# Key maxima and value sums of a block-sparse attention moved within set-up, with transposes ahead of them

## The chip, the core and the metric

The kernel runs on one core of a Trainium2 chip. The metric is the device time of one execution in microseconds, the median of three runs. Besides the program's span, from its first to its last instruction, an execution's time holds some 1.5 us around it. The engines are TensorE (PE), its weight load (PEld), VectorE (DVE), ScalarE (ACT), GpSimd (POOL) and SyncE (SP), which here only issues DMAs. TensorE's clock has two levels, 2.4 GHz (granted clock 1.00) and 1.2 GHz (0.50).

## The reference

Three stages follow each other: attention in 2 x 8 heads over 768 positions of width 64, a mixture of 8 experts with one expert per token, and a dense layer with a rational activation. Only the attention's set-up changes:

```python
block, window = (32, 16)
k_sum = k.reshape(B, H, nb, block, D).max(axis=3)      # block maxima of K
v_sum = v.reshape(B, H, nb, block, D).mean(axis=3)     # block means of V
scores_l = scale * np.matmul(q, k.transpose(0, 1, 3, 2))
mask_l = np.abs(pos[:, None] - pos[None, :]) < window
scores_s = scale * np.einsum('bhsd,bhnd->bhsn', q, k_sum) + np.log(block)
scores_all = np.concatenate([np.where(mask_l, scores_l, -1e9), scores_s], axis=-1)
a = softmax(scores_all)
out = np.matmul(a, np.concatenate([v, v_sum], axis=2))
```

Each position attends to the 31 keys around it and to the 24 block maxima of its head; the 24 block means of V stand beside the local values.

## The kernel before

Each engine runs its own program, written out by hand, and the programs meet in semaphores. An engine works in order, so a waiting instruction holds up all that is written behind it on its engine.

**Data.** 2 x 8 heads x 24 blocks make 384 block rows, three groups of 128 partitions (`KG` = 3). A row of `kraw` or `vraw` is one block of 32 positions x 64 elements, 1 MB per group. Groups 0 and 1 are needed for the first batch, group 2 with group 1 for the second.

**Set-up, keys.** SyncE loads `kraw` group by group (`load_k`, L366). ScalarE rounds each half of a group to the high part `KHL[HI]` (`key_halves`, L706), VectorE subtracts for the low part (`key_lo`, L964). TensorE transposes high and low side by side, four blocks of 128 columns per step, 8 steps per group, 24 in all (`key_columns`, L1341 is the line of every transpose). Step i writes bank i % 6, and may do so once step i - 6 has been copied out to `KTc`. ScalarE copies the steps (L713) but for steps 17, 19 and 21, which VectorE copies (`DVE_FILLS`, L970). VectorE makes the block maxima with a ladder of halving `max` operations over the row, in place in `kraw` (`key_max`, L977 the first step, L981 the four others), then splits the result into `KMX` (L983, L984). TensorE transposes `KMX` (`key_maxima`), ScalarE copies it to `KSs` (L717). Before, the maxima of groups 0 and 1 are made in set-up, those of group 2 in units 0 and 2 of the attention loop; TensorE's transpose of them stands at unit 4, into bank 7.

**Set-up, values.** TensorE sums each V group by matmuls with the identity into one bank (`value_sums`, L1357, banks 7 and 6), VectorE reduces the bank and scales (`mean_v`, L989, L990) and raises `vmean_ready`. SyncE stores the means to DRAM (L406), loads them back in the layout of `VA` (L402), and only then loads V's group 2 and query tile 2; GpSimd makes the third group's means with its own addition tree (`mean_v`, L522).

**Embedding.** ScalarE and VectorE normalise the expert embedding; TensorE transposes it; VectorE copies it (`place_embedding`, L957, L958), ahead of all its key work.

**GpSimd** makes `ident` (L472), then per query tile T: `split_q(T)` (high and low parts of the queries, L510 to L514) and `windows(T, half)` (gathers the keys of the tile from `KSs` and `KTc` into `KW`, L537, L539). `windows(0, 0)` waits for groups 0 and 1 of the columns and the first two maxima. Behind `windows(2, 1)` stand two loads of expert weights, the constants, and from tile 3 on, beside the tiles, the splitting of expert 0's weights in eight pieces (`split_slab0`, L549, L551: one piece with tile 3, two with 4, one with 5, two with 6, one each with 7 and 8) and indirect stores of x (L592).

**Attention loop.** 12 tiles x 4 head pairs = 48 units. Unit u on TensorE: `scores(u)` (L1424), `query_stack(u + 2)` (four transposes into bank 6 or 7), `transposes(u - 2)`, `products(u - 3)` (L1449, L1450). `query_stack(u)` with u % 4 == 0 waits for `split_q(u // 4)`. VectorE reduces scores to `es` (L1015) and copies `QS` for odd units (L1009), ScalarE does the exponentials (L742) and the even units' `QS` (L733).

The order of set-up on TensorE before:

```python
            embedding()
            key_columns(0)
            key_columns(1)
            key_maxima(0)
            value_sums(0)
            key_maxima(1)
            value_sums(1)
            key_columns(2)
```

## Time and profile before

| what | value |
|---|---|
| median of 3 runs (lowest, highest) | 752.04 us (751.38, 752.91) |
| the profiled execution: its time, its span | 747.03 us, 745.5 us |
| TensorE matmul busy | 684.3 us, 92% |
| VectorE, ScalarE, GpSimd busy | 500.2, 419.7, 171.9 us (67%, 56%, 23%) |
| chain that ended last, by engine | PE 76%, DMA 10%, DVE 5%, ACT 3% |
| mean granted TensorE clock | 0.97 |

The page cuts the span into 40 slices of 18.6 us; a digit is the busy share in tenths:

```profile
PE   4769999999387989999999999999999999999991
DVE  7576677676557468433411637899989899898881
POOL 4366999331331312111001000100000020200002
PEclk9989999999599999999999999999999999999997
```

The first three slices are set-up and the loop's first units, attention ends in the eleventh slice. TensorE is busy 4, 7 and 6 tenths there and 9 or more in the attention loop behind. GpSimd is nearly full in slices 5 to 7, and TensorE's clock is short of full in slice 3.

### The profile page before, as it was taken

Reading aid. Unit: us, or ns where it says so; the run is one execution under the profiler, and the core shown is the slowest. Engines: PE = TensorE matmul, PEld = TensorE weight load, DVE = VectorE, ACT = ScalarE, POOL = GpSimd, SP = SyncE. Lnnn points to the kernel's source line nnn. Section 1 sums busy time; section 2 is a strip of 40 time slices with the busy share of each in tenths; the row PEclk is TensorE's granted clock in tenths of the full one; section 3 lists DMA queues with packets and bytes.
Section 4 is the critical chain, followed back from the end, with each engine's and each line's share of the span. In section 5 each row is a group of like instructions: output and inputs, shape, how many; then the busy total and the mean of one; then the engine's idle time right before and its main releaser. Section 6 shows DMA issues by size and latency. Waiting matters only on the chain.

```text
span 745.5 us, 11775 instructions
## 1 busy us (share of the span) xinstructions
PE 684.3 (92%) x3397; PEld 547.3 (73%) x3397; DVE 500.2 (67%) x975; ACT 419.7 (56%) x786; POOL 171.9 (23%) x233
## 2 busy tenths in 40 slices
PE   4769999999387989999999999999999999999991
PEld 4457777777276777777888788888888888888871
DVE  7576677676557468433411637899989899898881
ACT  5445565565335577533523527777666666766650
POOL 4366999331331312111001000100000020200002
PEclk9989999999599999999999999999999999999997
DMA  8233544311698499823723440101000020100001
GB/s 295 56 93 113 135 131 109 79 47 45 212 325 252 139 308 323 276 59 105 265 84 100 142 157 15 57 0 30 15 14 1 1 71 1 42 15 1 0 1 56
DMA packets 52182, 77.75 MB, mean 104 GB/s; under 512 B 31680, under 2 KB 31696, under 8 KB 50840
## 3 DMA queue, kind: packets, MB, share of 16 engines
q1 hardware_dynamic: 43608, 51.51, 22.4%
q0 software_dynamic: 8064, 25.46, 10.3%
q8 instruction: 31, 0.51, 0.3%
q14 instruction: 31, 0.25, 0.1%
q10 hardware_dynamic: 448, 0.02, 0.1%
HBM read 63.50 MB, written 13.48 MB: 103 GB/s over the span
## 4 chain that ended last, share of the span: by engine, by line
PE 76%; DMA 10%; DVE 5%; ACT 3%; issue 2%; SPq 1%; POOL 1%; DVEq 1%; ACTq 0%; POOLq 0%
PE bank L1594 18%; PE bank L1609 17%; PE bank L1562 10%; PE bank L1341 10%; PE bank L1541 8%; DMA raw_late<-in_moe_w_dram 8%; PE bank L1450 4%; PE bank L1424 4%; PE bank L1449 3%; DVE weights L1206 2%; ACT weights L792 2%; DMA kraw<-in_k_dram 2%; PE bank L1469 1%; PE bank L1357 1%; DMA x_by_slot<-VA,zidx 1%
## 5 line engine op out<-in xcount | busy, mean ns | idle before, releaser
L1609 PE MATMUL bank<-weights,G 128*128 128x512 f32 x576 | 140.7, 393 | 1.9 <-DVE G L1206 1.9
L1594 PE MATMUL bank<-X2T,weights 128*128 128x512 f32 x576 | 141.1, 394 | 0.0
L1609 PEld LDWEIGHTS bank<-weights,G 128*128 128x128 f32 x576 | 108.1, 188 | 27.1 <-DVE G L1206 2.6
L1594 PEld LDWEIGHTS bank<-X2T,weights 128*128 128x128 f32 x576 | 107.5, 188 | 23.6
L1541 PE MATMUL bank<-weights,XT 128*128 (+1 forms) x456 | 116.9, 406 | 8.2 <-issue 4.0
L1562 PE MATMUL bank<-weights,HT 128*128 x456 | 112.6, 403 | 6.0 <-DVE HT L1206 6.0
L1541 PEld LDWEIGHTS bank<-weights,XT 128*128 128x128 f32 x456 | 85.3, 192 | 30.4 <-issue 11.8
L1562 PEld LDWEIGHTS bank<-weights,HT 128*128 128x128 f32 x456 | 85.7, 191 | 26.4 <-issue 7.1
L844 ACT ACTIVATE qd<-bank,coef 128x512 f32<-128x512 f32 x48 | 33.1, 689 | 73.5 <-PE bank L1594 73.4
L1206 DVE TENSOR_TENSOR HT<-bank,HT 128x512 fp32r<-128x512 f32 x38 | 24.5, 685 | 70.2 <-ACT HT L869 68.5
L742 ACT ACTIVATE es<-es,nmx 128x182 f32<-128x182 f32 x96 | 42.5, 444 | 25.5 <-DVE nmx L1015 25.5
L631 POOL DMA_DIRECT2D y_in_order<-yo x19 | 10.6, 557 | 200.2 <-ACT yo L896 200.2
L1206 DVE TENSOR_TENSOR weights<-raw_late,weights 128x2048 f32 (+1 forms) x20 | 41.4, 2077 | 22.4 <-ACT weights L792 22.4
L1206 DVE TENSOR_TENSOR weights<-raw_early,weights 128x2048 f32 (+2 forms) x20 | 40.6, 2075 | 15.5 <-ACT weights L792 15.2
L1256 DVE SCALAR_TENSOR_TENSOR qd<-sq,absb,qd 128x512 f32<-128x512 f32 x48 | 36.1, 751 | 21.1 <-ACT sq L845 21.1
L1015 DVE CUSTOM_DVE_ANT_0 es<-bank,mask 128x182 f32<-128x182 f32 x96 | 31.3, 344 | 22.5 <-PE bank L1424 22.0
L792 ACT CAST weights<-raw_late 128x2048 f32 x16 | 30.3, 1912 | 24.1 <-DMA raw_late<-in_moe_w_dram 24.1
L644 POOL DMA_INDIRECT out_dram<-ost,token_of x12 | 12.6, 1048 | 126.3 <-DVE ost L1244 123.3
L869 ACT CAST HT<-bank 128x512 fp32r<-128x512 f32 x38 | 20.4, 591 | 36.6 <-PE bank L1341 34.9
L852 ACT ACTIVATE pb<-bank,ncoef 128x512 f32<-128x512 f32 x48 | 37.9, 789 | 0.0
L1273 DVE SCALAR_TENSOR_TENSOR pb<-pb,ncoef,rr 128x512 f32<-128x512 f32 x48 | 36.1, 752 | 1.7
L1266 DVE SCALAR_TENSOR_TENSOR pb<-pb,ncoef,bank 128x512 f32<-128x512 f32 x48 | 35.9, 748 | 1.7
(215 smaller groups left out, 1156.1 us busy)
## 6 DMA issues: line engine op xcount, KB each, us to landing
raw_early<-in_moe_w_dram SPq DMA_DIRECT2D x14, 1024.0 KB, 8.2
raw_late<-in_moe_w_dram SPq DMA_DIRECT2D x14, 1024.0 KB, 10.3
y_in_order<-yo POOLq DMA_DIRECT2D x19, 256.0 KB, 3.2
x_all<-in_moe_w_dram POOLq DMA_DIRECT2D x8, 512.0 KB, 3.9
kraw<-in_k_dram SPq DMA_DIRECT2D x3, 1024.0 KB, 8.3
qraw<-in_q_dram SPq DMA_DIRECT2D x12, 256.0 KB, 4.1
x<-y_in_order POOLq DMA_DIRECT2D x12, 256.0 KB, 3.1
VA<-in_v_dram SPq DMA_DIRECT2D x10, 208.0 KB
```

Source lines behind the costliest of these rows:

```text
L742: A_.activation(e_, e_, ACT.Exp, bias=nmx[:, slot:slot + 1], scale=-1.0, accum_out=sums[:, T % 2, 2 * p + i:2 * p + i + 1]).then_inc(exp_d ...
L792: A_.copy(W[:, bass.ds(other, 1), HI, c * CH:(c + 1) * CH].rearrange("p s n -> p (s n)"), raw[c]).then_inc(half_hi[c // PER], 1)
L852: A_.activation(pb[s], h, ACT.Identity, bias=ncoef[:, 2:3], scale=ncoef[:, 3:4]).then_inc(lin_done, 1)
L1206: return V.tensor_tensor(out_, src, hi.bitcast(F32), ALU.subtract)
L1256: V.scalar_tensor_tensor(q_, h2, absb[:, 1:2], q_, ALU.mult, ALU.add).then_inc(q_done, 1)
L1266: V.scalar_tensor_tensor(g_, g_, ncoef[:, 1:2], h, ALU.add, ALU.mult).then_inc(h_read, 1)
L1273: V.scalar_tensor_tensor(g_, g_, ncoef[:, 0:1], r_, ALU.add, ALU.mult).then_inc(g_sb, 1)
L1341: return T_.transpose(dst, src, ident[0:rows, 0:rows])
L1541: last = T_.matmul(bank[half][:, :], XT[:, xa, kc * P:(kc + 1) * P], weights(par, wa, kc * F + half * BANK), start=(kc == 0 and n_ == 0), ...
L1562: last = T_.matmul(bank[5][:, :], HT[:, ha, fc * P:(fc + 1) * P], weights(par, wa, KC * F + fc * DM), start=(fc == 0 and n_ == 0), stop=(f ...
L1594: last = T_.matmul(bank[6 + f % 2][:, :], W[:, 0, wa, kc * F2 + f * P:kc * F2 + (f + 1) * P], X2T[c % 2][:, xa, kc * C_TOK:(kc + 1) * C_TO ...
L1609: last = T_.matmul(bank[tt][:, :], G[:, f % 2, ga, tt * P:(tt + 1) * P], W[:, 1, wa, f * DM:(f + 1) * DM], start=(f == 0 and n_ == 0), sto ...
```

## The change

SyncE issues the load of K's group 2 ahead of both V groups. VectorE's ladder for group 0 is no longer split around `key_lo(1)`, and the maxima of group 2 are made in set-up, behind `mean_v(0)` and ahead of the three key columns that VectorE copies; `mean_v(1)` goes behind those. All three maxima are transposed into bank 6, both value sums use bank 7 (so the second waits for `vmean_ready` 1), and TensorE's order becomes: 36 transposes of the identity into bank 7, embedding, 16 more, key columns 0 and 1, maxima 0, value sums 0, maxima 1, key columns 2, value sums 1, maxima 2. `query_stack(0)` waits for the third maxima's copy, `query_stack(1)` for the second means, and the loop for all 24 columns. ScalarE copies ten steps before it rounds group 2 instead of eight. The maxima leave the loop on all engines.

```diff
--- before.py
+++ after.py
@@ -408,9 +408,9 @@
             load_k(0)
             load_k(1)
             load_q(0)
+            load_k(2)
             load_v_all(0)
             load_v_all(1)
-            load_k(2)
             load_q(1)
             sp.wait_ge(cleared, 1)
             load_v(0)
@@ -706,25 +706,26 @@
                     A_.copy(KHL[:, g % 2, rows, HI, :],
                             kraw[:, g, :].rearrange("p (r d) -> p r d", d=D)[:, rows, :]).then_inc(k_hi, 1)
 
-            def key_columns(g):
-                for i in range(g * FILLS, (g + 1) * FILLS):
+            def key_columns(first, end):
+                for i in range(first, end):
                     if i not in DVE_FILLS:
                         act.wait_ge(kt_mm, i + 1)
                         A_.copy(kt_dst(i), kt_src(i)).then_inc(kt_act, 1)
 
             def key_maxima(g):
                 act.wait_ge(ks_mm, g + 1)
-                A_.copy(KSs[:, g * P:(g + 1) * P], bank[(6, 6, 7)[g]][:, g % 2 * P:(g % 2 + 1) * P]).then_inc(ks_sb, 1)
+                A_.copy(KSs[:, g * P:(g + 1) * P], bank[6][:, g * P:(g + 1) * P]).then_inc(ks_sb, 1)
 
             norm_of_embedding()
             key_halves(0)
             key_halves(1)
-            key_columns(0)
+            key_columns(0, FILLS + 2)
             key_halves(2)
-            key_columns(1)
+            key_columns(FILLS + 2, 2 * FILLS)
             key_maxima(0)
             key_maxima(1)
-            key_columns(2)
+            key_columns(2 * FILLS, KG * FILLS)
+            key_maxima(2)
 
             def query_stack(u):
                 act.wait_ge(q_mm, u + 1)
@@ -772,8 +773,6 @@
                     copy_pt(u - 2)
                 if u < UNITS:
                     exponent(u, 1)
-                if u == 4:
-                    key_maxima(2)
                 if u % 4 in (0, 2) and 4 <= u < UNITS + 4:
                     out_half(u // 4 - 1, u % 4 // 2)
                 if u % 4 == 1 and 9 <= u:
@@ -969,38 +968,34 @@
                 dve.wait_ge(kt_mm, i + 1)
                 V.tensor_copy(kt_dst(i), kt_src(i)).then_inc(kt_dve, 1)
 
-            def key_max(g, first, last):
+            def key_max(g):
                 t = kraw[:, g, :]
                 dve.wait_ge(k_lo, 2 * g + 2)
-                if first:
-                    w = ROW // 2
+                w = ROW // 2
+                while w >= D:
                     link(V.tensor_tensor(t[:, 0:w], t[:, 0:w], t[:, w:2 * w], ALU.max))
-                if last:
-                    w = ROW // 4
-                    while w >= D:
-                        link(V.tensor_tensor(t[:, 0:w], t[:, 0:w], t[:, w:2 * w], ALU.max))
-                        w //= 2
-                    link(V.tensor_copy(KMX[:, g, HI, :], t[:, 0:D]))
-                    V.tensor_tensor(KMX[:, g, LO, :], t[:, 0:D], KMX[:, g, HI, :].bitcast(F32), ALU.subtract)\
-                     .then_inc(kmax_ready, 1)
+                    w //= 2
+                link(V.tensor_copy(KMX[:, g, HI, :], t[:, 0:D]))
+                V.tensor_tensor(KMX[:, g, LO, :], t[:, 0:D], KMX[:, g, HI, :].bitcast(F32), ALU.subtract)\
+                 .then_inc(kmax_ready, 1)
 
             def mean_v(g):
                 dve.wait_ge(vm_mm, g + 1)
-                link(V.tensor_reduce(vmean[:, g, :], bank[7 - g][:, :].rearrange("p (r d) -> p d r", d=D), AX.X, ALU.add))
+                link(V.tensor_reduce(vmean[:, g, :], bank[7][:, :].rearrange("p (r d) -> p d r", d=D), AX.X, ALU.add))
                 V.tensor_scalar(vmean[:, g, :], vmean[:, g, :], 1.0 / BLOCK, None, ALU.mult).then_inc(vmean_ready, 1)
 
             scale_embedding()
             place_embedding()
             key_lo(0)
-            key_max(0, True, False)
             key_lo(1)
-            key_max(0, False, True)
-            key_max(1, True, True)
+            key_max(0)
+            key_max(1)
             key_lo(2)
             mean_v(0)
-            mean_v(1)
+            key_max(2)
             for i in DVE_FILLS:
                 key_column(i)
+            mean_v(1)
 
             def query_stack(u):
                 dve.wait_ge(q_mm, u + 1)
@@ -1112,8 +1107,6 @@
                     query_stack(u + 2)
                 if u % 4 in (0, 2) and 4 <= u < UNITS + 4:
                     out_half(u // 4 - 1, u % 4 // 2)
-                if u in (0, 2):
-                    key_max(2, u == 0, u == 2)
                 if u % 4 == 3 and u >= 7 and u < LOOPS - 1:
                     make_x(u // 4 - 1)
 
@@ -1352,9 +1345,9 @@
             def value_sums(g):
                 pe.wait_ge(v_all_in[g], 16)
                 if g == 1:
-                    pe.wait_ge(ks_sb, 2)
+                    pe.wait_ge(vmean_ready, 1)
                 for j in range(4):
-                    last = T_.matmul(bank[7 - g][:, :], ident[:, :], vraw[g][:, j * BANK:(j + 1) * BANK],
+                    last = T_.matmul(bank[7][:, :], ident[:, :], vraw[g][:, j * BANK:(j + 1) * BANK],
                                      start=(j == 0), stop=(j == 3))
                 last.then_inc(vm_mm, 1)
 
@@ -1377,21 +1370,25 @@
                 if g == 1:
                     pe.wait_ge(ks_sb, 1)
                 if g == 2:
-                    wait_qs(pe, 5)
-                transpose(bank[(6, 6, 7)[g]][:, g % 2 * P:(g % 2 + 1) * P], KMX[:, g, :, :].rearrange("p a d -> p (a d)").bitcast(F32))\
+                    pe.wait_ge(ks_sb, 2)
+                transpose(bank[6][:, g * P:(g + 1) * P], KMX[:, g, :, :].rearrange("p a d -> p (a d)").bitcast(F32))\
                     .then_inc(ks_mm, 1)
 
+            def warm_up(n):
+                for _ in range(n):
+                    transpose(bank[7][:, 0:P], ident[:, :])
+
+            warm_up(36)
             embedding()
+            warm_up(16)
             key_columns(0)
             key_columns(1)
             key_maxima(0)
             value_sums(0)
             key_maxima(1)
+            key_columns(2)
             value_sums(1)
-            key_columns(2)
-            wait_fills(pe, KG * FILLS)
-            pe.wait_ge(vmean_ready, 2)
-            pe.wait_ge(ks_sb, 2)
+            key_maxima(2)
 
             def query_stack(u):
                 T, p = divmod(u, PAIRS)
@@ -1401,8 +1398,10 @@
                     wait_qs(pe, u - 2)
                 if u % 4 == 2 and u >= 10:
                     pe.wait_ge(x_done, (u - 10) // 4 + 1)
-                if u == 7:
+                if u == 0:
                     pe.wait_ge(ks_sb, KG)
+                if u == 1:
+                    pe.wait_ge(vmean_ready, 2)
                 if u % 4 == 3 and u >= 11:
                     pe.wait_ge(lg_read, (u - 11) // 4 + 1)
                 for i in range(2):
@@ -1491,9 +1490,8 @@
 
             query_stack(0)
             query_stack(1)
+            wait_fills(pe, KG * FILLS)
             for u in range(LOOPS):
-                if u == 4:
-                    key_maxima(2)
                 if u % 4 == 0 and u >= 8:
                     if u >= 12:
                         if PAIRS * (u // 4 - 2) + 9 < UNITS:
```

## Rows read from the trace of the kernel before

**Rows 1.** Chain of waits, from the start: start us, length us, what.

```profile
5.79 14.17 DMA kraw<-in_k_dram
...
39.74 1.19 DVE kraw L977
```

**Rows 2.** Timeline of TensorE: start us, us, line, what, times [idle before it].

```profile
7.71 0.56 PE L1341 MATMUL bank<-ident,x_all 8*128 8x8 f32 x4 [7.71 <-DVE x_all L951]
10.08 8.79 PE L1341 MATMUL bank<-ident,KHL 128*128 128x128 f32 x56 [1.81 <-DVE KHL L964]
22.52 1.97 PE L1341 MATMUL bank<-ident,KHL 128*128 128x128 f32 x8 [3.64 <-ACT KTc L713]
...
29.11 3.67 PE L1357 MATMUL bank<-x_all,ident 128*128 128x512 f32 x8 [0.45 <-ACT KSs L717]
...
38.33 0.69 PE L1424 MATMUL bank<-KW,QS 128*128 128x182 f32 x4 [0.24 <-ACT QS L733]
...
50.49 0.44 PE L1341 MATMUL bank<-ident,KMX 128*128 128x128 f32 x1 [5.57 <-DVE QS L1009]
```

**Rows 3.** Timeline of VectorE.

```profile
15.56 2.81 DVE L981 TENSOR_TENSOR kraw<-kraw 128x512 f32<-128x512 f32 x4
...
20.03 1.74 DVE L981 TENSOR_TENSOR kraw<-kraw 128x512 f32<-128x512 f32 x4
...
28.59 0.69 DVE L989 TENSOR_REDUCE vmean<-bank 128x64 f32<-128x512 f32 x1 [4.07 <-PE bank L1357]
...
33.54 0.67 DVE L990 TENSOR_SCALAR vmean<-vmean 128x64 f32<-128x64 f32 x1
...
46.91 2.30 DVE L984 TENSOR_TENSOR KMX<-kraw,KMX 128x64 fp32r<-128x64 f32 x1
```

**Rows 4.** Windows: stretch, busy us (instructions) per engine, granted clock, DMA share, GB/s.

```profile
10.00:11.00 1.00, 0.92 (x5) 0.92 (x6) 1.00 (x2) 1.00 (x2) 0.00 (x0) 1.00 0.52 108
15.00:16.00 1.00, 1.00 (x11) 1.00 (x10) 1.00 (x2) 0.82 (x3) 1.00 (x1) 1.00 1.04 434
...
22.50:25.40 2.90, 2.88 (x11) 2.37 (x12) 2.02 (x2) 2.90 (x7) 0.00 (x0) 0.50 0.28 51
...
50.50:59.30 8.80, 8.80 (x32) 6.85 (x33) 3.20 (x13) 3.97 (x15) 7.74 (x22) 0.50 0.51 156
```

**Rows 5.** Timeline of SyncE's DMA issues.

```profile
2.43 2.56 SPq L371 DMA_DIRECT2D vraw<-in_v_dram  x1
...
37.00 0.42 SPq L377 DMA_DIRECT2D qraw<-in_q_dram  x1
```

**Rows 6.** DMA issues, 0 to 30 us: KB each, median us from issue to landing.

```profile
vraw<-in_v_dram SPq DMA_DIRECT2D x1, 1024.0 KB, 12.4
```

**Rows 7.** Timeline of GpSimd.

```profile
1.50 0.28 POOL L472 TENSOR_SCALAR_AFFINE_SELECT ident<-ident 128x128 f32<-128x128 f32 x1 [0.25 <-POOL ident L475]
...
14.53 2.25 POOL L514 TENSOR_TENSOR qhl<-qraw,qhl 128x512 fp32r<-128x512 f32 x1
...
42.82 0.61 POOL L510 CAST qhl<-qraw 128x512 fp32r<-128x512 f32 x1 [7.78 <-DMA qraw<-in_q_dram]
...
63.21 0.27 POOL L537 CAST KW<-KSs 128x96 fp32r<-128x96 f32 x1 [1.93 <-PE bank L1424]
63.42 0.71 POOL L539 CAST KW<-KTc 128x632 fp32r<-128x632 f32 x1
...
111.64 1.26 POOL L514 TENSOR_TENSOR qhl<-qraw,qhl 128x512 fp32r<-128x512 f32 x1
```

**Rows 8.** Instructions on tile kraw: duration ns min/median/max, first and last start us.

```profile
L964 DVE TENSOR_TENSOR KHL<-kraw,KHL x6: 1218/1222/1632, 8.8 to 23.3; 128x1024 fp32r<-128x1024 f32 x6
```

**Rows 9.** Timeline of TensorE, unit 26.

```profile
118.43 0.60 PE L1341 MATMUL bank<-ident,qhl 128*128 128x128 f32 x4
```

**Rows 10.** What TensorE waited for, 60 to 190 us: total, times, longest.

```profile
PE bank L1485 <- DVE oh L1068: 1.0, 1, 1.0
PE bank L1469 <- ACT OT L755: 0.4, 1, 0.4
```

## The prediction

> **What bounds the kernel now.** I read the page first, then the chain of waits, then each engine's timeline over the first 62 us, then the granted clock in windows of the same stretch. Through the attention loop the chain is TensorE's almost alone, so time saved in set-up reaches the end only if nothing else in the loop is nearly as late. The diff touches set-up and the loop's first steps; everything behind the loop is ordered by waits on its end, so I pass a shift on one for one.
>
> The start of the chain shows the two places the edit touches. K's third group lands at 5.79 + 14.17 = 19.96 us, behind both V groups [rows 1], and TensorE is idle from 18.87 (10.08 + 8.79) to 22.52. V's sums then run as one block, key columns follow, and the first scores come at 38.33 [rows 2]. In units 0 and 2 VectorE does the third group's maxima inside the loop; the last step ends at 46.91 + 2.30 = 49.21 [rows 3]. TensorE idles 5.57 us for it and restarts at 50.49 [rows 2]. It restarts slow: the granted clock is 0.50, the 1.2 GHz level, up to 59.3 at least [rows 4]. One trap: from 10 to 11 us the clock reads 1.00, the 2.4 GHz level, yet only 5 matmuls ran, and 11 in the us from 15 [rows 4]. The array was in fact slow until about 15 us, 4.9 us after the work at 10.08 began.
>
> **The loop's stall, the known gain.** With the maxima in set-up the loop loses the 5.57 us, the first maxima step in the chain (1.2, at 39.74), and what half clock costs: 8.8 us at half rate do the work of 4.4 [rows 1, 2, 4]. That is 11.2 us on TensorE's side, all on the path.
>
> **Load order.** The first V group, issued at 2.43, landed 12.4 later, at 14.8 [rows 5, 6]; K's third came 5.1 after that with one group between. The groups have one size and one queue, so I exchange the places: K's third at 14.8, V at 17.4 and 20.0. Nobody needs V before 19 (below). Cost nothing.
>
> **Warm-up.** The 36 transposes start when ident is ready, 1.78 [rows 7]. At half clock eight transposes took 1.97, some 0.22 each less the last one's tail [rows 2]; at full clock half of that. So they end at 9.7 all slow, 5.7 all fast, 8.2 with the rise after 4.9 us. The embedding's transposes started at 7.71 [rows 2], and VectorE's key work queues behind the copies that wait for them: 0 to 2 us on VectorE's chain, I take 0.5. The 16 later ones (1.8 us) fit before the first KHL halves. What warm-up brings is that the first 64 key transposes run at 0.11. They then are done well before VectorE has the maxima, so this gain is hidden.
>
> The Trainium skill (TensorE: Matmul & The Clock Gate, Part 4: PE-mode transpose) says that transposes don't count as work for the clock; the warm-up would do nothing. The trace disagrees: from 10.08 to 18.87 TensorE did transposes only, and their rate doubled near 15 [rows 2, 4]. By that rule the time would be the third rival's.
>
> **VectorE's chain decides set-up.** Up to the end of the second group's maxima its work is only permuted, and was without a gap; it ended 22.26, now 22.8. Then come, in the new order: key_lo(2), two of 1.22 [rows 8], to 25.2; mean_v(0), 0.93 (28.59 to 29.52) [rows 3], for which V's first sums (3.67 us [rows 2], from about 19.1) are on time; key_max(2), whose ladder takes 1.2 + 1.74 and the KMX steps 0.5, 3.4 clean [rows 1, 3]. Clean it ends at 29.5. But GpSimd works beside it. Beside its query split (its subtraction 2.25 instead of 1.26 us [rows 7]) VectorE's key_lo took 1.63 each instead of 1.22, the ladder 2.81 instead of 1.74, 1.9 us in all, and one 0.23 us step beside GpSimd's addition 2.30 [rows 3, 8]. In the new order GpSimd gets its key sums at about 23.4 and does windows(0), split_q(1), windows(1): two pairs of 0.27 and 0.71 for each windows [rows 7], about 1.9, and 2.4 for the split, 6.2 in all, in the time of key_lo(2) and key_max(2). For split_q I take 1.9 as before, for the windows 0.7 of their 3.8. So key_max(2) ends at 32.1; bounds 29.5 and 35.7.
>
> The Trainium skill (SBUF — State Buffer, Who interferes with whom) says that a VectorE operation with two SBUF inputs and a GpSimd operation that reads SBUF exclude each other for the whole instruction. The 2.30 us step agrees. By that rule the upper bound is nearer and the time up to 3.6 us longer.
>
> **The new wait.** TensorE's transposes of key group 2 start at about 23.9 and reach step 23, whose bank VectorE's column 17 frees. That column now queues behind key_max(2). It takes 0.7, so TensorE stands from about 27.0 to 32.8; queued behind are step 23, V's second sums, the third maxima's transpose and the query stacks. 5.8 us idle: after gaps of 3.64 and 5.57 the clock was down at the restart [rows 2, 4], so it is here. The slow spells after work began were 2.9, 4.9 and 8.8 us; I take 4.9, half clock until 37.7. Step 23 is 0.85, to 33.6. V's second sums are 3.67 warm; 4.1 us at half rate do 2.05 of it, 1.6 are left: 39.3 (38.3 with 2.9, 40.9 with 8.8). Then mean_v(1), 0.9: vmean_ready 2 at 40.2. It was 33.54 + 0.67 = 34.21 [rows 3]: **6.0 us later**. query_stack(1) waits for it, so the first scores come at about 41.3, 3.0 later than 38.33. TensorE alone would gain 11.2 - 3.0 = 8.2.
>
> **Who else hangs on vmean_ready.** SyncE stores the means, loads them back, and only then loads V's third group and the third query tile, at 37.00, 2.8 us after vmean_ready 2 [rows 5]; it lands at 42.82, and GpSimd sat idle 7.78 us for it [rows 7]. Behind it on GpSimd lie split_q(2), windows(2), the addition tree over V's third group, two DMA issues, the constants and split_q(3). All of that moves 6.0 later, less 0.6 as VectorE's ladder no longer slows split_q(2) (3.1 us against 2.5). GpSimd waited for TensorE 1.93 us before windows(3, 1) [rows 7] and twice more like it, 4.9 in all; these waits go as TensorE comes earlier. split_q(7) ended at 111.64 + 1.26 = 112.90; now at 112.9 + 5.4 - 4.9 = 113.4. TensorE took that tile up at 118.43 [rows 9], and between 60 and 190 us it waited once for VectorE (1.0), once for ScalarE (0.4), for GpSimd never [rows 10]. The slack was 5.5, so TensorE can come at most 5.5 - 0.5 = **5.0 us** earlier at this place. GpSimd becomes the loop's bound and cuts 8.2 to 5.0; behind tile 7 it issues less work per tile and has slack again.
>
> The sum: the profiled execution took 747.03 with a span of 745.5; the new span is 740.5. The runs' median is 752.04, 5.0 above the profiled one, so I forecast 752.0 - 5.0 = 747.0.
>
> **Rivals.** (1) Little contention, or no fall of the clock: maxima end at 30.0, then 0.7 + 0.4 + 3.7 + 0.9 give vmean_ready 2 at 35.7, 1.5 late; GpSimd's bound is 5.5 + 4.9 - (1.5 - 0.6) = 9.5, the time 742.5. For it: clean durations; against: rows 3. (2) Half clock reaches into the loop: the 8.8 us spell speaks for it, the two shorter ones against. If 8.8 us lie in the loop, TensorE loses 4.4 of its 8.2: 748.2, with later sums too up to 750. (3) Warm-up does nothing: 64 key transposes at 0.22 from 11.8 end at 25.9, V's first sums at about 31, mean_v(0) waits for them, key_max(2) ends near 36.5, V's second sums at 44.7, vmean_ready 2 at 45.6, 11.4 late: gain 10.4 - 10.8 = -0.4, time 752.4. Against: the rate that doubled near 15. (4) Slower: half clock stays on in the loop, whose hand-offs are short gaps for TensorE. It costs half of its length, and TensorE has 8.2 in hand: from 16.4 us of half clock nothing is gained, from 19.4 it is slower by over 0.2%, 26 us give 756.8. For: the spell from 50.49 lasted 8.8 us though TensorE was never idle; against: no spell was half as long as this needs. (5) The gain is lost later, in the expert stage's weight loads: 752; against: their issue waits for attention's end, so they move along.
>
> **Chances.** Forecast case 0.50 (own range 745.2 to 748.8, vmean_ready 2 between 38.4 and 42); (1) 0.22; (2) 0.12; (3) 0.06; (4) 0.05; (5) 0.05. The range takes in (1) and (2): 741.8 to 750.6. Faster by over 0.2% 0.84, within 0.2% 0.08 (case 5 and half of 3), slower 0.08. 0.2% is 1.5 us, about what a measurement of this kernel can tell from no change.
>
> **What would show it.** K's third group landing near 14.8; 11 matmuls per us from 10 us on; a gap of TensorE of 5 to 6 us ended by a VectorE key column, with the clock at 0.50 behind it; the second vmean scaling ending near 40 and the third query tile landing near 49; no idle of TensorE in units 3 and 4; waits of TensorE's query transposes for GpSimd's split at tile 7. I am wrong if key_max(2) ends near 30, or if TensorE waits for GpSimd nowhere: then the gain is 8 to 11.

## The result: slower by 0.6%, with a new stall in unit 6

The forecast was 5.0 us faster, with a range that reached to 1.4 us faster at its upper end. Measured over twelve runs of each kernel on one chip, the kernel after takes 753.91 us in the median and the kernel before 749.88; the ratio is 1.0062, 95% interval 1.0035 to 1.0089, which is 2.6 to 6.7 us slower.

The profiled execution of the kernel after took 758.35 us with a span of 756.8, 11.3 above the profiled one of before. SyncE's first issue behind its wait for attention's last products splits this. The first fence is from the kernel before, the second from the kernel after; both are SyncE's timeline (start us, us, what).

```profile
186.36 0.91 SPq L436 DMA_DIRECT2D raw_early<-in_moe_w_dram  x2
```

```profile
192.98 0.90 SPq L436 DMA_DIRECT2D raw_early<-in_moe_w_dram  x2
```

Attention ends 6.6 us later. The stretch behind it has the same code in both and took 559.1 us before and 563.8 after; over the profiles of the other twelve kernels of this study it took 555.9 to 562.4, and the medians differ by 4.0 us and not by 11.3, so I put the other 4.7 us down to scatter. "Attention's end" below is the start of this row. It comes from one profiled execution of each kernel, while the ratios come from all the timed ones.

The page of the kernel after, busy tenths in 40 slices of 18.9 us:

```profile
PE   8686999999387998989999999999999999999991
DVE  7743666766457557532331445899989899898881
POOL 4446899530331113110011000100000020100002
PEclk9895999999789999999999999999999999999997
```

TensorE fills the first slice better than before (8 tenths against 4: the warm-up), but in slice 4, from 57 to 76 us, it is at 6 and its clock at 5, where before both were at 9. VectorE is at 3 there. TensorE's rows in slices 2 to 4:

```profile
32.47 1.09 PE L1334 MATMUL bank<-ident,KHL 128*128 128x128 f32 x4 [5.96 <-DVE KTc L969]
...
33.35 5.27 PE L1350 MATMUL bank<-x_all,ident 128*128 128x512 f32 x8
...
40.68 0.66 PE L1423 MATMUL bank<-KW,QS 128*128 128x182 f32 x4 [0.39 <-ACT QS L734]
...
63.87 1.22 PE L1448 MATMUL bank<-PT,VA 128*128 128x256 f32 x2 [8.35 <-DVE PT L1018]
```

The 5.57 us of [rows 2] at 50.49 are gone. The new wait in set-up is there as forecast, 5.96 us at 32.47. And there is one nobody forecast: 8.35 us until 63.87, for VectorE's copy of PT. (PT is the transposed copy of the exponentials, which the products read.) The timelines of VectorE, ScalarE and GpSimd show what held that copy:

```profile
52.52 0.08 DVE L1010 DVE_READ_ACCUMULATOR2_ANT nmx<- 128x1 f32 x1
62.78 0.17 DVE L1090 COPY bank<-iota_e 128x8 f32<-128x8 f32 x1 [10.18 <-POOL tri L472]
...
63.13 0.69 DVE L1018 COPY PT<-bank 128x512 f32<-128x512 f32 x1
```

```profile
63.25 0.45 ACT L743 ACTIVATE es<-es,nmx 128x182 f32<-128x182 f32 x1 [9.65 <-DVE nmx L1010]
```

```profile
48.17 0.61 POOL L510 CAST qhl<-qraw 128x512 fp32r<-128x512 f32 x1 [16.52 <-DMA qraw<-in_q_dram]
...
51.40 5.43 POOL L522 TENSOR_TENSOR vraw<-vraw 128x1024 f32<-128x1024 f32 x5
...
62.39 0.29 POOL L472 TENSOR_SCALAR_AFFINE_SELECT tri<-tri 128x64 f32<-128x64 f32 x1
```

In units 6 and 7 VectorE writes a row of indices beside the scores, for the routing. It waits for the constants that GpSimd makes:

```python
                if u in (6, 7):
                    dve.wait_ge(consts_ready, 1)
                    V.tensor_copy(bank[u % 2][:, IOTA:IOTA + E], iota_e[:, 1, :])
```

`tri` is the last constant and raises `consts_ready`. Before, the same copy ran at 61.0 us, 3.0 after `tri` had ended at 58.06, without a wait:

```profile
L1095 DVE COPY bank<-iota_e x2: 164/165/166, 61.0 to 63.6; 128x8 f32<-128x8 f32 x2
```

After, the loop reaches it 8.4 us earlier (at 52.60), and `tri` ends 4.6 later (at 62.68), as its queue stood behind a query tile that landed 5.35 later (48.17 against 42.82 [rows 7]). 8.4 + 4.6 - 3.0 = 10.0; the row says 10.18. Behind VectorE's wait stood the unit's second score reduction, so ScalarE's exponential, the next copy of PT, and TensorE. The windows from there (stretch, busy us and instructions of PE, PEld, DVE, ACT, POOL, granted clock, DMA share, GB/s), after and then before:

```profile
58.00:63.90 5.90, 0.03 (x1) 0.03 (x1) 1.08 (x5) 0.65 (x3) 5.21 (x17) 0.50 0.88 224
63.90:77.00 13.10, 13.10 (x46) 9.92 (x46) 6.51 (x26) 4.62 (x16) 8.25 (x11) 0.50 0.34 88
78.00:80.00 2.00, 2.00 (x16) 1.67 (x15) 1.19 (x7) 0.85 (x3) 0.84 (x2) 1.00 0.00 0
```

```profile
63.90:77.00 13.10, 13.10 (x87) 9.78 (x86) 8.54 (x35) 8.47 (x29) 9.68 (x13) 1.00 0.46 108
```

Behind the stall the clock is at its lower level until about 77.7 us. TensorE is never idle in the 13.1 us and gets 46 matmuls done instead of 87. The sum: TensorE's own gain is 11.2 - 2.35 (first scores 40.68 instead of 38.33 [rows 2]) = 8.85; it pays 8.35 for the stall and half of 13.8 us, 6.9, for the clock. -8.85 + 8.35 + 6.9 = 6.4 later, measured 6.6.

The kernel before took up the same products, those of unit 4, here (its timeline of TensorE):

```profile
63.85 0.60 PE L1449 MATMUL bank<-PT,VA 128*128 128x256 f32 x2
```

63.85 us before, 63.87 after: the stall ate what TensorE had gained and no more, and the kernel falls behind only in the 13.8 us that follow.

### The profile page after: what moved, and what is told of

The parts are those of the page before. It is cut to its first block, busy times and chain, and to the rows that moved or that the text cites. A ratio compares the mean times of both kernels' runs of the same rounds, so it can differ in the third digit from the quotient of the medians.

```text
span 756.8 us, 11876 instructions
## 1 busy us (share of the span) xinstructions
PE 694.7 (92%) x3449; PEld 554.4 (73%) x3449; DVE 498.8 (66%) x975; ACT 419.2 (55%) x786; POOL 173.6 (23%) x233
## 3 DMA queue, kind: packets, MB, share of 16 engines
q1 hardware_dynamic: 43608, 51.51, 21.9%
## 4 chain that ended last, share of the span: by engine, by line
PE 74%; DMA 10%; DVE 7%; ACT 3%; POOL 2%; issue 2%; DVEq 1%; SPq 0%; ACTq 0%; POOLq 0%
PE bank L1592 18%; PE bank L1607 17%; PE bank L1560 10%; PE bank L1334 9%; PE bank L1539 8%; DMA raw_late<-in_moe_w_dram 8%; PE bank L1449 4%; PE bank L1423 3%; PE bank L1448 3%; DVE weights L1199 2%; ACT weights L791 2%; DVE kraw L976 2%; PE bank L1468 2%; DVE KHL L963 1%; DMA qraw<-in_q_dram 1%
## 5 line engine op out<-in xcount | busy, mean ns | idle before, releaser
L631 POOL DMA_DIRECT2D y_in_order<-yo x19 | 10.6, 557 | 203.2 <-ACT yo L895 203.2
L868 ACT CAST HT<-bank 128x512 fp32r<-128x512 f32 x38 | 20.5, 591 | 36.3 <-PE bank L1334 34.7
L1448 PE MATMUL bank<-PT,VA 128*128 128x256 f32 x96 | 30.3, 399 | 8.3 <-DVE PT L1018 8.3
```

Source lines behind the costliest of these rows:

```text
L1448: T_.matmul(O_, VA[:, r, p * P:(p + 1) * P], PT[:, u % 2, 0:2 * P], start=True, stop=False)
```

## The experiments

The theory: the wait for `consts_ready` turns the gain into a loss, in two parts of about equal size (the stall, and half clock behind it), and it arises since TensorE reaches unit 6 earlier while the new set-up raises `vmean_ready` to 2 later (39.59 instead of 34.21) and with it the query tile ahead of the constants. Rivals: the stall is a symptom and what comes next is as late (GpSimd's query split); the loss is set-up's (the 5.96 us gap); half clock comes from the loop and not from the stall. All kernels below compute the whole reference. Each comparison was made against runs of the kernel before on the same chip, so ratios are compared, not medians.

### The constants moved ahead of the query tiles

The block from `upper` to `tri` goes on GpSimd from behind `load_raw(1)` to the front, where GpSimd later sits idle for its query tile anyway.

```diff
             G_.memset(es[:, :, 2 * KEYS:3 * P + KB], 0.0)
+            link(G_.memset(upper[:, :], 1.0))
...
+            keep_where(tri[:, :, :], ALU.is_ge, 0, [[1, E], [-1, E]], 0, 0.0).then_inc(consts_ready, 1)
             split_q(0)
```

> The changed kernel with GpSimd's block of constants (which ends in consts_ready) moved to the start, behind the memset of es, where GpSimd is idle for 7.8 us. Theory A: the loss is VectorE's wait for consts_ready in unit 6 (10.18 us idle at 62.78) and the half clock behind it. Then that wait is gone, TensorE has no gap of 8 us in the loop, and the time is some 10 us under the changed kernel and about 6 us under the kernel before (ratio to before 0.992). Rival B: GpSimd's work per tile or the late query tile is the bound: then the constants are worth at most their own 3.0 us, ratio to before about 1.002. Rival C: the loss lies behind attention: no change, ratio 1.006.

Measured: ratio 0.9891 (0.9849 to 0.9933), attention's end 179.07, 13.9 earlier than after and 7.3 earlier than before. Set-up is that of after (`vmean_ready` 2 at 39.63), the copy runs at 52.57 without a wait, and from 40 to 90 us the clock is never below full. TensorE waits once for GpSimd (its timeline):

```profile
111.06 0.66 PE L1334 MATMUL bank<-ident,qhl 128*128 128x128 f32 x4 [0.67 <-POOL qhl L514]
```

Moving work that takes 3.1 us (59.60 to 62.68 in the kernel after) turns the change from slower into faster by 1.1%, so the wait for it was what lost the gain. The rival, that something else is just as late, holds for 0.67 us only: that is the bound the forecast had named, GpSimd's split at tile 7. Of TensorE's gain of 8.85 us, 7.3 arrive, and 0.67 is this wait. The scores of unit 8 start 8.4 us earlier than before (57.88 against 66.31), those of unit 24 8.2 and those of unit 27 7.3. So 0.4 is missing from the start (the 11.2 were some 0.4 too many), 0.2 goes at unit 11, and the rest is lost around this wait.

The same move in the kernel before:

> The kernel before with the same move of GpSimd's constants. Its VectorE reaches unit 6 at 61.0, 3.2 us after consts_ready, and never waited for it. Theory A: no change, ratio 1.000 within noise. Rival B (GpSimd's chain is already nearly the bound): up to 3 us faster, ratio 0.996.

Ratio 0.9995 (0.9966 to 1.0025), attention's end 187.34 against 186.36. There the constants' place costs nothing: the slack of 3.0 us was real. The loss is made by the change and this place together.

### The consumer moved instead of the producer

```diff
-                if u in (6, 7):
+                if u in (8, 9):
```

> The changed kernel with GpSimd's program untouched and only VectorE's two copies of the iota rows, with their wait for consts_ready, moved from units 6 and 7 to units 8 and 9, ahead of their first reader. Theory A: VectorE comes to the wait 6 us later, so it lasts about 2 us and not 10, TensorE's gap is too short for the clock to fall, and the time is 7 to 9 us under the changed kernel (ratio to before 0.994 to 0.997). Rival B: nothing on GpSimd has moved, so the loop still waits for it: ratio 1.006 as changed.

Ratio 0.9942 (0.9911 to 0.9973), attention's end 181.51. The wait is shorter and still there (VectorE's timeline, then TensorE's):

```profile
62.12 0.17 DVE L1090 COPY bank<-iota_e 128x8 f32<-128x8 f32 x1 [3.87 <-POOL tri L472]
```

```profile
62.84 1.07 PE L1334 MATMUL bank<-ident,qhl 128*128 128x128 f32 x4 [2.54 <-DVE lgw L1047]
```

Two units are 5.1 us, too few against 10.2. With the producer where it was, the stall of 2.54 and a short spell of low clock (3.4 us) leave this kernel 2.4 us behind the one above, although its set-up happened to run 0.8 faster (first scores at 39.93). It confirms the pair as cause from the other side.

### The stall kept, the clock held

What share is the stall's own, and what share the clock's? 72 transposes of the identity into bank 4, which is free there, fill the stall; the one wait put in is one that the next products have anyway.

```diff
+            def keep_busy(n):
+                wait_ot(pe, 1)
+                for _ in range(n):
+                    transpose(bank[4][:, 0:P], ident[:, :])
...
+                if u == 7:
+                    keep_busy(72)
```

> The changed kernel with 72 more transposes of the identity on TensorE in unit 7, in the place where it stands idle for 8.35 us, into a bank that is free. The wait for the constants stays; only what TensorE does in it changes. Theory: the granted clock stays 1.00 and the 14 us at 0.50 behind the stall go, which gives back 7 us less what the fillers overrun (under 1 us): ratio to before 0.997 to 0.999. Rival: the half clock costs little since other engines bound the units anyway: ratio 1.006.

Ratio 0.9987 (0.9957 to 1.0016), attention's end 186.42. VectorE's wait stands at 10.14 us, as in the kernel after, and TensorE's real work resumes at 63.65 against 63.87. TensorE's timeline and the window behind it:

```profile
55.18 8.02 PE L1334 MATMUL bank<-ident 128*128 128x128 f32 x72
63.65 0.70 PE L1448 MATMUL bank<-PT,VA 128*128 128x256 f32 x2 [0.44 <-DVE PT L1018]
```

```profile
63.90:77.00 13.10, 13.10 (x84) 9.68 (x84) 9.30 (x39) 8.69 (x29) 12.46 (x18) 1.00 0.44 108
```

84 matmuls instead of 46 in the same window. Attention ends 6.56 earlier than after with the stall in full: that is the clock's share, 6.9 by the sum above. The stall's own share is 186.42 - 179.07 = 7.35. With the stall alone the change is even (186.42 against 186.36 before), so both are needed for a slower kernel.

### The gap in set-up

VectorE's three key columns stand behind the third maxima, and TensorE waits 5.96 us for the first of them. ScalarE makes them here, all 24:

```diff
-        DVE_FILLS = (2 * FILLS + 1, 2 * FILLS + 3, 2 * FILLS + 5)
+        DVE_FILLS = ()
```

> The changed kernel with the three key columns that VectorE copies (17, 19, 21) given to ScalarE (DVE_FILLS empty), which sits idle from 27 to 33 us. Theory A: step 23 no longer waits for VectorE's maxima, V's second sums end near 31 and vmean_ready 2 comes near 32.6 in place of 39.6; the query tile, the constants and the loop's start all move 7 us earlier together, the wait in unit 6 stays about 8 to 10 us long. Time 7 us under the changed kernel, ratio to before about 0.997. If the chain over vmean_ready isn't what delays the constants, the wait in unit 6 grows instead and the gain is near 0.

`vmean_ready` 2 comes at 32.55 instead of 39.59 and the first scores at 34.06 instead of 40.68, but attention's end (186.38) is only 6.6 earlier than after and the time that of before, ratio 0.9993 (0.9962 to 1.0024). The wait in unit 6 is still 7.45 us. The constants come 6.4 us earlier, but the loop reaches them only 3.7 earlier (48.88 instead of 52.60), since TensorE's clock is at 0.50 for 6.8 us from 33.5 on, at the start of the loop:

```profile
56.33 0.17 DVE L1090 COPY bank<-iota_e 128x8 f32<-128x8 f32 x1 [7.45 <-POOL tri L472]
```

```profile
57.41 1.22 PE L1448 MATMUL bank<-PT,VA 128*128 128x256 f32 x2 [5.61 <-DVE PT L1018]
```

Both edits at once:

> The changed kernel with both edits: constants at GpSimd's start and the three key columns given to ScalarE. If the wait for the constants and the wait of step 23 are two costs that add, the loop starts 6 to 7 us earlier as with the second edit alone (first scores 34.1) and runs without the wait in unit 6 as with the first. TensorE then asks for query tile 7 at 34.1 + (118.43 - 38.33 - 11.2) = 103.0; GpSimd, whose query tile 2 comes 6.5 us earlier, ends split_q(7) near 105, so GpSimd is the bound by some 2 us. Time 12 to 14 us under the kernel before, ratio 0.982 (0.979 to 0.986). Rival: GpSimd was already the bound with the constants moved alone (one wait of 0.7 us at tile 3 there), then ratio stays near 0.989.

Ratio 0.9778 (0.9731 to 0.9825), 732.52 us beside 748.83: the best kernel of the study, 16.3 us below before, and better than both kernels of the change. Attention's end is 172.18, 6.9 us earlier than with the constants' move alone, as the first scores come 6.8 earlier (33.85). The ratio lies below the expected 0.979 to 0.986. The expectation had GpSimd as the bound by some 2 us; TensorE does not wait for it once, but asks for query tile 7 only 0.3 us after it is ready (104.3 against 103.99), so this kernel has reached that bound. So what set-up loses at the gap (its 5.96 us and the half clock behind it) is passed on one for one, once the loop has no other wait; in the kernel after, most of it only changed who waits.

In this kernel too the clock fell, behind a gap of 1.42 us (30.15 to 31.57) and hand-offs of 0.45 and 0.16 (TensorE's timeline, then the window):

```profile
31.57 0.33 PE L1334 MATMUL bank<-ident,KMX 128*128 128x128 f32 x1 [1.42 <-DVE KMX L979]
...
33.85 1.13 PE L1423 MATMUL bank<-KW,QS 128*128 128x182 f32 x4 [0.16 <-issue]
```

```profile
33.00:36.00 3.00, 2.84 (x15) 2.47 (x13) 1.31 (x5) 0.71 (x2) 0.00 (x0) 0.50 0.38 65
```

### Warm-up and load order, each undone

`warm_up(36)` and `warm_up(16)` taken out of the kernel after, and out of the best kernel:

> The changed kernel without its 36 + 16 transposes of the identity. Theory: VectorE's chain decides set-up, the slow array up to 15 us hides behind it and ScalarE's copies; key transposes take 3 us longer but the step-23 gap and the start of the loop move by under 0.6 us. Ratio to before 1.006 as changed, within noise. Rival: the warm-up is worth its 25 slow transposes (2.7 us): ratio 1.010.

> Both edits without the 52 transposes of the identity. VectorE's chain starts 8.8 either way and still decides: it had no gap up to the third maxima. Key transposes of groups 0 and 1 end near 20 in place of 17.5 and V's first sums near 23.6, before VectorE wants them (24.4). Ratio to before as with the warm-up, 0.978 within 0.001. Rival: now that the hidden time is shorter, the slow array shows: 1 to 2.5 us, ratio 0.980 to 0.981.

From after: ratio 1.0060 (1.0026 to 1.0093), attention's end 192.87 against 192.98. From the best: 0.9815 (0.9790 to 0.9839), 172.10 against 172.18. The second was expected at 0.978 within 0.001; its interval overlaps that of the best kernel (0.9731 to 0.9825). In the first, the transposes of groups 0 and 1 take 10.08 us instead of 7.57, and nobody waits for them (without warm-up, then after; TensorE's timeline):

```profile
10.10 10.08 PE L1334 MATMUL bank<-ident,KHL 128*128 128x128 f32 x64 [1.82 <-DVE KHL L963]
```

```profile
1.83 6.16 PE L1334 MATMUL bank<-ident 128*128 128x128 f32 x36 [1.83 <-POOL ident L472]
...
10.14 7.57 PE L1334 MATMUL bank<-ident,KHL 128*128 128x128 f32 x64
```

The warm-up does what it is for. Windows of the kernel after (columns as above):

```profile
3.00:4.00 1.00, 1.00 (x6) 1.00 (x5) 0.17 (x1) 0.29 (x1) 0.78 (x2) 1.00 0.84 340
6.00:7.00 1.00, 1.00 (x11) 1.00 (x10) 0.64 (x5) 0.86 (x2) 0.00 (x0) 1.00 0.94 304
```

The granted clock reads 1.00 in both, but 6 transposes of the identity ran in the one and 11 in the other. The faster array is worth nothing here, neither alone nor with the other two edits. From the best kernel the first scores even come 0.4 us earlier without it (33.42): TensorE's gap ahead of the third maxima is 0.90 instead of 1.42, and the clock stays at 1.00. That this does not show at attention's end fits GpSimd as the bound: TensorE waits 1.1 us for GpSimd's query splits there.

K's third group back behind V's two:

```diff
-            load_k(2)
             load_v_all(0)
             load_v_all(1)
+            load_k(2)
```

> The changed kernel with K's third group loaded behind both V groups, as before. It lands near 20 us in place of 15; ScalarE's halves of it end near 22 in place of 18.9, and its six columns near 25 in place of 21.8, so the key sums, GpSimd's windows and the low halves come up to 3 us later. VectorE is busy with maxima until 22, so I expect the maxima's end, vmean_ready 2 and the loop at most 1 us later: ratio 1.006 to 1.008. Rival: the load order is what makes the early set-up possible: 3 us later, ratio 1.010.

A miss. Ratio 1.0002 (0.9969 to 1.0035) and attention's end 189.29, 3.7 earlier than after, although the group lands later (19.8 instead of 15.3). VectorE's ladder and TensorE's gap:

```profile
25.22 3.77 DVE L976 TENSOR_TENSOR kraw<-kraw 128x1024 f32<-128x1024 f32 x5
```

```profile
30.86 0.63 PE L1334 MATMUL bank<-ident,KHL 128*128 128x128 f32 x4 [2.51 <-DVE KTc L969]
31.32 3.60 PE L1350 MATMUL bank<-x_all,ident 128*128 128x512 f32 x8
```

The ladder takes 3.77 instead of 5.05, since GpSimd's windows start later (25.74 instead of 23.04) and overlap less of it; TensorE's work ahead of the gap is later (it waits 2.46 us at 24.98 for ScalarE, whose queue stands behind the late group), so the gap is 2.51 instead of 5.96, the clock holds at 1.00 behind it, and V's second sums take 3.60 instead of 5.27. `vmean_ready` 2 comes at 35.88. The earlier load brought TensorE sooner to a place where it has to wait longer.

Is it then always better? In the best kernel:

> Both edits with K's third group loaded behind V, as before. Without VectorE's columns step 23 no longer waits, so the contention on VectorE's ladder costs only its own 1.3 us and no fall of the clock: theory D says the load order is then worth 0 to 1.5 us, ratio to before 0.976 to 0.978. Rival: the old order is 4 us better here too, ratio 0.972.

Another miss, to the other side: 0.9839 (0.9804 to 0.9873) against 0.9778 (0.9731 to 0.9825), intervals that touch; in the profiled executions attention's end is 179.35 against 172.18. K's third group landed at 21.9 in this one, ScalarE stood for it with the copies of the first maxima behind, TensorE waited for ScalarE, and its clock fell:

```profile
27.13 0.45 PE L1334 MATMUL bank<-ident,KMX 128*128 128x128 f32 x1 [4.96 <-ACT KSs L717]
27.37 6.04 PE L1334 MATMUL bank<-ident,KHL 128*128 128x128 f32 x32
```

So as far as these two pairs show, the load order has no price of its own. Its worth is the length of the gap that TensorE meets, and whether the clock falls in it.

### VectorE and GpSimd side by side

`windows(0, 0)` on GpSimd waits for the third maxima, so that the ladder runs alone:

```diff
             split_q(0)
+            pool.wait_ge(kmax_ready, KG)
             windows(0, 0)
```

> The changed kernel (K's third group ahead of V, as changed) with one wait added on GpSimd: windows(0) starts only when VectorE has the third maxima (kmax_ready 3). It tests why the old load order was faster. Theory D: with K's third group early, GpSimd's windows and split_q(1) run beside key_max(2) and stretch its ladder from 3.0 to 5.05 us, so the gap before step 23 is 5.96 us and the clock falls. Then here the ladder is 3.0 us again, the gap 4 us or less, V's second sums 3.6 us if the clock holds, vmean_ready 2 near 35.5 to 37 in place of 39.6, and the ratio to before 1.000 to 1.002. Rival E: the early load's transfers themselves or the order on ScalarE cost it: ladder short but vmean_ready 2 still near 39, ratio 1.006.

The first fence is VectorE's timeline of this kernel, the second that of after:

```profile
25.84 2.99 DVE L977 TENSOR_TENSOR kraw<-kraw 128x1024 f32<-128x1024 f32 x5
```

```profile
25.79 5.05 DVE L976 TENSOR_TENSOR kraw<-kraw 128x1024 f32<-128x1024 f32 x5
...
31.11 0.61 DVE L979 TENSOR_TENSOR KMX<-kraw,KMX 128x64 fp32r<-128x64 f32 x1
```

Alone the five steps take 2.99 us, beside GpSimd 5.05. The maxima end at 29.31 instead of 31.72 and the gap is 2.90 instead of 5.96. The clock falls behind it all the same, for some 3.4 us from 31.2, so V's second sums take 5.30 us and not the 3.6 expected; `vmean_ready` 2 comes at 36.79 instead of 39.59, and attention's end at 187.19 instead of 192.98. The timed ratio is 1.0052 (1.0032 to 1.0072), against 1.0062 of after, while the profiled execution's attention ends within 0.8 us of that of before, which would be 1.001, the upper end of what was expected being 1.002. The contention and its size are shown by the rows; what its removal brings in time I could not settle. Added to the best kernel:

> Both edits (constants early, three key columns on ScalarE) and that wait on GpSimd. The third maxima end 2 us earlier, near 29.6 in place of 31.6, and vmean_ready 2 with them, 30.8 if V's second sums (done near 30.2) allow it; but GpSimd's windows(0) then come only near 31.5, which the first scores (33.9 before this edit) need. Theory D: 1 to 2 us faster than with both edits alone, ratio to before 0.976. Rival: GpSimd's later start eats it, ratio 0.978 or above.

0.9826 (0.9790 to 0.9861) against 0.9778, intervals that overlap, attention's end 172.16 against 172.18. `vmean_ready` 2 comes 1.0 earlier (31.36), and TensorE spends it waiting (what TensorE waited for, 40 to 190 us: total, times, longest):

```profile
PE bank L1335 <- POOL qhl L514: 2.3, 2, 1.5
```

GpSimd's chain is no earlier than in the best kernel: the query tile is asked for 1.0 us earlier (34.15 instead of 35.13) but lands at 41.01, against 40.90 there. Here this chain is the bound, and a faster set-up has nothing more to give as long as it stands.

## Why the prediction was wrong, step by step

**Right, by its own rows.** K's third group was to land at 14.8 and landed at 15.3. Warm-up was to end at 8.2 and to cost VectorE 0.5; it ended at 7.99 and VectorE's key work began at 8.86 against 8.8 before. The third maxima were to end at 32.1 (31.72), with the ladder slowed by GpSimd; the clean end, 29.5, is what the runs without GpSimd beside it showed (29.31). TensorE's gap at step 23 was to be 5.8 (5.96) and at half clock up to 37.7; the windows have the higher level again within the us from 36. V's second sums were to end at 39.3 (38.6), `vmean_ready` 2 at 40.2 (39.59), the first scores at 41.3 (40.68), the third query tile at 49 (48.17). Units 3 and 4 have no stall.

**The step that failed** is "Who else hangs on vmean_ready". It followed the late query tile through GpSimd's queue and named the constants in it, as time that GpSimd spends, and went on to split_q(3). It did not ask who waits for the constants. The forecast had both terms: TensorE 8.2 earlier, GpSimd's queue behind the tile 5.4 later, and the copy's slack of 3.0 could be read. 8.2 + 5.4 - 3.0 = 10.6 is the wait, measured 10.18. VectorE would then be 5.4 - 3.0 = 2.4 later than before at this place, and the one clock spell in the loop that the profile had, 8.8 us [rows 4], gives 4.4 more: 6.8 later, near the measured 6.6, but by luck. The stall alone leaves attention's end even with before (186.42 against 186.36) and not 2.4 later: VectorE restarts 1.8 us later (62.78 against 61.01), but before, its copy of PT was ready (61.50 + 0.69 = 62.19) 1.7 us ahead of the products at 63.85, and that slack takes it up. The clock cost 6.6 instead of 4.4. The kind of wait was looked for (a consumer that comes earlier, a producer that comes later), but only at TensorE's own waits [rows 10], and TensorE waits for this one through two other engines.

**GpSimd as the bound at tile 7** was right as a mechanism and hidden by the earlier stall. In the kernel after, TensorE waits for GpSimd nowhere, which the prediction had named as a sign of a gain of 8 to 11 us; it came with a loss. split_q(7) ends at 119.49 instead of the 113.4 forecast. With the constants ahead it ends at 111.00 and TensorE waits 0.67 for it. The cap of 5.0 on the gain becomes 5.0 + 3.1 = 8.1 with the constants out of the way; TensorE reached the tile at 111.06 instead of 118.43 [rows 9], 7.4 earlier.

**Load order, "cost nothing",** was half right. Nobody missed V. But in the kernel after the earlier group made the set-up gap 3.4 us longer (5.96 against 2.51) and let the clock fall, 3.7 us of attention's time lost; where the later load opened a gap of its own, in the best kernel, the earlier one was worth 7.2 of attention's time in the profiled executions. The step asked who needs the moved load and not where those that it hurries will stand.

**Rivals.** The fourth names the outcome, and half clock in the loop, but neither its cause nor, by its own price, its size. It put half clock down to short hand-offs and called the kernel slower from 19.4 us on. The windows from 40 to 90 us add up to 20.5, but 6.7 of them lie inside the stall, where TensorE had nothing to run; the 13.8 behind it cost 6.9, less than the 8.2 in hand. It took the stall as well, and the run with the clock held shows that the spell belongs to it. The first is refuted by the 5.05 us ladder and the clock at 0.50 behind the gap, the second by the clock, back within the us from 36, ahead of the first scores at 40.68, the fifth by the medians, which differ by 4.0 us where attention's end already differs by 6.6, the third by the warm-up's windows. The Trainium skill (TensorE: Matmul & The Clock Gate, Part 4: PE-mode transpose) has transposes not counted as work for the clock; here 36 of them brought the full rate and 72 of them kept the clock at 1.00 through a stall, so the measurement decides against that sentence. The rule of the Trainium skill (SBUF — State Buffer, Who interferes with whom), that VectorE's operations with two SBUF inputs and GpSimd's reads exclude each other, agrees with the ladder in direction, 5.05 us beside GpSimd against 2.99 alone. It is no full exclusion here: in the same 5.0 us GpSimd did work that takes it 3.3 without the ladder beside it (48.17 to 51.43), and 2.99 + 3.3 is more than 5.0.

## What to carry to other kernels

When a semaphore's increment moves, in place or in time, list every wait on it on every engine, with the slack of each in the trace of before; do the same for each instruction queued behind a late transfer, down to the last constant. Where a stage gets faster, look at what it used to reach late enough: a wait that never showed in a profile has only a slack, and 3.0 us of it decided 14 us here. Price each stall of TensorE twice, once for its length and once for the low clock behind it, and compare kernels by the gap that remains and by the clock behind it, not by how early the work ahead of it ran.

## What the runs showed of the hardware that was not expected

The clock's part of a stall was nearly as large as the stall: 6.6 us behind one of 8.35, and 13.8 us of continuous work passed before the higher level came back, against the 2.9 to 8.8 us of the kernel before. The length of a gap alone does not tell whether the clock falls. Behind gaps of 0.90 and 2.51 us it stayed at 1.00. Behind gaps of 1.42 (with key columns on ScalarE and the constants early), 2.54 and 2.90 us it fell for some 3.4 us each, behind one of 1.41 (key columns on ScalarE alone) for 6.8, and it fell behind 4.96 and 5.96 too. What decides between them no run here shows.

GpSimd pays for sharing as well. Its query split beside VectorE's ladder, GpSimd's timeline of the kernel after, and the same line without VectorE's ladder beside it:

```profile
27.90 1.69 POOL L514 TENSOR_TENSOR qhl<-qraw,qhl 128x512 fp32r<-128x512 f32 x1
...
118.23 1.26 POOL L514 TENSOR_TENSOR qhl<-qraw,qhl 128x512 fp32r<-128x512 f32 x1
```

The same load can land 2 us apart: K's third group in the old order came at 19.8 and at 21.9 us in two kernels with the same queue ahead of it; in the second TensorE's gap was 4.96 us.
